# Two squared tiles per chunk in two halves, the low part as the third pass, and T3 ahead of y

## The reference, cut to what matters

```python
# attention: pooled keys/values, softmax, weighted sum -> x (12288 tokens x 128)
# layer 1 (128 -> 2048 -> 128)
h = x @ w_in1; r = np.maximum(h, 0.0); g = r * r
x2 = g @ w_out1
# layer 2 (128 -> 2048 -> 128)
h = x2 @ w_in2
P = a[0] + a[1]*h + a[2]*h**2 + a[3]*h**3
Q = 1.0 + np.abs(b[0])*np.abs(h) + np.abs(b[1])*h**2
out = (P / (Q + 1e-06)) @ w_out2
```

## Time and profile before

| | |
|---|---|
| median of 3 runs | 1517.82 us (1517.7 to 1518.0) |
| profiled execution, its own time | 1517.89 us |
| its span | 1515.9 us |
| granted TensorE clock, mean | 1.0 |
| PE, DVE, ACT, POOL busy | 98%, 95%, 91%, 82% |

### The profile page before, as it was taken

How to read it: one execution, slowest core, us unless ns; L and a number is a source line. 1 busy time by engine, 2 the same in 40 slices (tenths; PEclk the granted TensorE clock), 3 DMA queues, 4 the chain that set the end, 5 groups by cost and what they waited for, 6 DMA issues and landing times.

```text
span 1515.9 us, 20584 instructions
## 1 busy us (share of the span) xinstructions
PE 1483.7 (98%) x5576; PEld 991.1 (65%) x5576; DVE 1445.2 (95%) x2549; ACT 1378.8 (91%) x2672; POOL 1248.3 (82%) x1225
## 2 busy tenths in 40 slices
PE   5999999999999999999999999999999999999988
PEld 4999999765666666666666666666666666666655
DVE  7888888889999999999999999999999999999998
ACT  3777777689999999999999999999999999999997
POOL 4544445359999999999999999999999999999897
PEclk9999999999999999999999999999999999999999
DMA  6200001000000000000000000000000000000000
GB/s 224 84 21 28 21 27 43 1 1 1 8 8 8 1 8 8 8 8 1 7 8 8 0 8 8 8 1 8 7 8 1 8 8 8 8 1 8 8 8 7
DMA packets 11518, 24.21 MB, mean 16 GB/s; under 512 B 1440, under 2 KB 2336, under 8 KB 11168
## 3 DMA queue, kind: packets, MB, share of 16 engines
q1 hardware_dynamic: 11424, 23.14, 4.5%
HBM read 16.85 MB, written 6.29 MB: 15 GB/s over the span
## 4 chain that ended last, share of the span: by engine, by line
PE 88%; DVE 5%; ACT 2%; POOL 2%; issue 1%; DMA 1%; SPq 0%; POOLq 0%; ACTq 0%; DVEq 0%
PE psum L937 19%; PE psum L974 18%; PE psum L801 11%; PE psum L800 11%; PE psum L802 11%; PE psum L889 6%; PE psum L852 6%; PE psum L874 4%; DVE tb L727 1%; DVE tb L736 1%; DVE tb L753 1%; DVE g1h L713 1%; DVE psum L741 1%; POOL tb L410 1%; DMA X<-kvT 1%
## 5 line engine op out<-in xcount | busy, mean ns | idle before, releaser
L412 POOL TENSOR_TENSOR wb<-wb,ub 128x512 f32<-128x512 f32 x384 | 496.4, 1293 | 29.4
L937 PE MATMUL psum<-tb,wout 128*128 128x512 f32 x736 | 375.8, 592 | 2.5 <-DVE tb L785 2.3
L974 PE MATMUL psum<-g,wout 128*128 128x512 f32 x690 | 352.4, 592 | 0.2 <-ACT x2f L528 0.2
L404 POOL TENSOR_SCALAR wb<-ub,babs 128x512 f32<-128x512 f32 x384 | 296.0, 771 | 35.5 <-ACT ub L550 30.3
L800 PE MATMUL psum<-x2h,win2h 128*128 128x512 f32 x384 | 283.3, 738 | 2.6 <-POOL x2l L397 2.5
L727 DVE SCALAR_TENSOR_TENSOR tb<-tb,ca,psum 128x512 f32<-128x512 f32 x364 | 267.8, 736 | 4.6 <-ACT psum L584 4.5
L736 DVE SCALAR_TENSOR_TENSOR tb<-tb,ca,psum 128x512 f32<-128x512 f32 x365 | 269.6, 739 | 0.0
L551 ACT ACTIVATE tb<-psum,ca 128x512 f32<-128x512 f32 x384 | 267.1, 696 | 0.0
L550 ACT ACTIVATE ub<-psum 128x512 f32<-128x512 f32 x384 | 233.0, 607 | 23.5 <-PE psum L802 23.5
L568 ACT ACTIVATE lnb<-wb 128x512 f32<-128x512 f32 x384 | 248.3, 647 | 5.2 <-POOL wb L412 4.8
L753 DVE SCALAR_TENSOR_TENSOR tb<-psum,tb 128x512 f32<-128x512 f32 x364 | 248.1, 682 | 2.6
(11 more groups left out here) (109 smaller groups left out, 2506.6 us busy)
## 6 DMA issues: line engine op xcount, KB each, us to landing
qraw<-qT SPq DMA_DIRECT2D x23, 256.0 KB, 2.6
outT<-osb SPq DMA_DIRECT2D x23, 256.0 KB, 2.0
X<-kvT SPq DMA_DIRECT2D x15, 384.0 KB, 7.7
wraw<-w_in SPq DMA_DIRECT2D x2, 1024.0 KB, 8.3
X<-kvT SPq DMA_DIRECT2D x2, 192.0 KB, 10.5
outT<-osb SPq DMA_DIRECT2D x2, 128.0 KB, 1.8
qraw<-qT SPq DMA_DIRECT2D x1, 192.0 KB, 10.2
wsr<-w_sr SPq DMA_DIRECT2D x1, 64.0 KB, 1.8
```

The source lines that it names most:

```text
L404: nc.gpsimd.tensor_scalar(w, u, babs[:, 1:2], babs[:, 0:1], ALU.mult, ALU.add).then_inc(v_rdy, 1)
L412: nc.gpsimd.tensor_tensor(w, w, u, ALU.mult).then_inc(w_rdy, 1)
L937: mm(ACC2, wout2[:, f, :], tb[:, t % T_RING, :], start=(f == 0), stop=(f == NF - 1))\
L974: mm(ACC1, wout1[:, f, :], g1[:, t % G_RING, :], start=(f == 0), stop=(f == NF - 1))\
```

## The change

Four edits. `SPLIT_COLS` gets column 5, so that two tiles per chunk go through the three-pass form: on each added tile PE does three fp32r passes in place of the f32 matmul, ACT makes one more high half (step 6) and POOL one more low half (end of step 5). POOL's `x1_high` moves from step 5 to step 6 and `x1_low` from step 5 to step 8. In `in2` and in `out1` of halved tiles the pass that reads the low part of the moving operand becomes the third, and the wait for that part stands right before it. On DVE, T3 (tile s-20) is issued ahead of y (tile s-21), except where POOL makes the T2 that T3 reads; both loops share this order.

```diff
-        SPLIT_COLS = (13,)
+        SPLIT_COLS = (5, 13)
...
             for s in range(STEPS):
-                if s % NF == 5 and 1 <= s // NF < NCH - 1:
+                if s % NF == 6 and 1 <= s // NF < NCH - 1:
                     x1_high(s // NF + 1)
+                if s % NF == 8 and 1 <= s // NF < NCH - 1:
                     x1_low(s // NF + 1)
...
-            for s in range(TAIL_S):
-                t = s - LAG - 2
+            def make_y(t):
+
                 if in_b(t):
                     y, r = tb[:, t % T_RING, :], h2(t)
                     dve.wait_ge(r_rdy, t + 1)
                     nc.vector.scalar_tensor_tensor(out=y, in0=y, scalar=ca[:, 0:1], in1=r,
                                                    op0=ALU.add, op1=ALU.mult).then_inc(y_rdy, 1)
-                t = s - LAG - 1
+
+            def make_t3(t):
+
                 if in_b(t):
                     p = tb[:, t % T_RING, :]
                     if by_pool(t):
@@ -735,6 +738,14 @@
                         dve.wait_ge(t2_rdy, t + 1 - pool_t2(t + 1))
                     nc.vector.scalar_tensor_tensor(out=p, in0=p, scalar=ca[:, 1:2], in1=h2(t),
                                                    op0=ALU.add, op1=ALU.mult).then_inc(t3_rdy, 1)
...
+            for s in range(TAIL_S):
+                if by_pool(s - LAG - 1):
+                    make_y(s - LAG - 2)
+                    make_t3(s - LAG - 1)
+                else:
+                    make_t3(s - LAG - 1)
+                    make_y(s - LAG - 2)
...
             for s in range(TAIL_S, STEPS):
-                t = s - LAG - 2
-                if in_b(t):
-                    y, r = tb[:, t % T_RING, :], h2(t)
-                    dve.wait_ge(r_rdy, t + 1)
-                    nc.vector.scalar_tensor_tensor(out=y, in0=y, scalar=ca[:, 0:1], in1=r,
...
+                if by_pool(s - LAG - 1):
+                    make_y(s - LAG - 2)
+                    make_t3(s - LAG - 1)
+                else:
+                    make_t3(s - LAG - 1)
+                    make_y(s - LAG - 2)
...
                     if t % NF == 0:
-                        pe.wait_ge(*((x2l0_rdy, 1) if c == 0 else (x2_rdy, c)))
+                        pe.wait_ge(x2h_rdy, c + 1)
...
-                    three(h2(t), win2h[:, f:f + P], win2l[:, f:f + P],
-                          x2h[:, c % 2, :], x2l[:, c % 2, :]).then_inc(h2_rdy, 1)
+                    mm(h2(t), win2h[:, f:f + P], x2h[:, c % 2, :], start=True, stop=False)
+                    mm(h2(t), win2l[:, f:f + P], x2h[:, c % 2, :], start=False, stop=False)
+                    if t % NF == 0:
+                        pe.wait_ge(*((x2l0_rdy, 1) if c == 0 else (x2_rdy, c)))
+                    mm(h2(t), win2h[:, f:f + P], x2l[:, c % 2, :], start=False, stop=True).then_inc(h2_rdy, 1)
...
                         pe.wait_ge(sqh_rdy, n + 1)
+                        mm(ACC1, wo1h[:, f, :], g1h[:, n % 2, :], start=(f == 0), stop=False)
+                        mm(ACC1, wo1l[:, f, :], g1h[:, n % 2, :], start=False, stop=False)
                         pe.wait_ge(sql_rdy, n + 1)
-                        three(ACC1, wo1h[:, f, :], wo1l[:, f, :], g1h[:, n % 2, :], g1l[:, n % 2, :],
-                              start=(f == 0), stop=(f == NF - 1)).then_inc(g1_used, 1)
+                        mm(ACC1, wo1h[:, f, :], g1l[:, n % 2, :], start=False, stop=(f == NF - 1)).then_inc(g1_used, 1)
```

## The result

The changed kernel takes 1525.55 us (median of 6 runs, 1525.02 to 1525.88), the kernel before 1517.92 us in runs beside it (1517.7 to 1518.12). The ratio is 1.005, 95% interval 1.0037 to 1.0063: slower by 7.6 us. Forecast was slower by 4.2 us, with a range that ended at 1525.2; the time lies 0.35 us above it.

A forecast was written before the change was run, and what follows sets the result against it. PE bounds the kernel before; after the change a loop over ACT and POOL does, at 49.91 us a chunk. 5.1 us for the chunks, less 0.4 and 0.5, give +4.2: 1522.0 us, forecast's own range 1519.5 to 1525.2, overall from 1513.3.

The forecast's parts named there:

- the sum behind the loop: Whole kernel: 21 rounds x 0.25 = 5.3 us, 5.1 with chunk 23, less 0.4 and 0.5 at the ends: +4.2 us.
- the last loop: Where the last loop opens, Exp waits 0.6 us for T3 once; T3 first takes 0.5 us off, between 0 and 0.6.
- the way in: Start of layer 2, before the 21 counted rounds: the prediction's sum has no term for it.
- a loop over ACT and POOL: Steady chunks: POOL's bursts delay ACT and ACT delays POOL, without PE; 49.91 us a chunk against PE's 49.50 and today's 49.66.
- four crossings: Where the round passes between ACT and POOL: into POOL at v(5) and v(13), back to ACT at Ln(11) and Ln(15).
- The stretches of the loop: One chunk's round from Abs(5): 21.00 us to Ln(11), 4.61 to Abs(13), 7.44 to Ln(15), 16.86 to Abs(5); together 49.91.
- The opening: Where layer 2 opens, two passes run before the wait for x2l: 0.4 us off, between 0 and 0.5.
- PE's saving: Each of 23 new halved tiles takes PE 0.15 us less, 3.5 us in all; PE's own work becomes 49.50 us a chunk.
- The first: Rival: PE stays the bound in the steady part, and 4.4 us come off, giving 1513.5 us; chance 0.15.
- Rival 3: More than the loop: PE stalls for x2l or out1 too, some 0.15 us a chunk more, 1525 us; chance 0.05.
- Rival 2: The loop lands near today's pace, 49.6 to 49.75 us a chunk, giving 1516 to 1519 us; chance 0.20.
- Rival 4: The halved tiles save PE nothing; given no chance of its own.

The follow-up runs named there:

- split5_only: The kernel before with column 5 halved as well and nothing else changed; x1_high and x1_low both stay at step 5: 1526.03 us, ratio 1.0053.
- no_split5: The changed kernel with column 13 alone halved; the move of x1_high and x1_low, the pass order and T3 first stay: 1516.82 us, ratio 0.9993.
- x1_at_3_7: The changed kernel with x1_high at step 3 instead of 6 and x1_low at step 7 instead of 8: 1514.46 us, ratio 0.9978.
- x37_y_first: The kernel x1_at_3_7 with the old order on VectorE, y ahead of T3, in both loops: 1515.59 us, ratio 0.9985.
- third_only: The kernel before with the low part as the third pass and its wait behind the first two passes, nothing else: 1517.56 us, ratio 0.9998.

## Why the prediction was right in kind and short in size

**The step that failed is the sum behind the loop: 21 rounds at 0.25 us, nothing for the way into them, and 0.5 us off for the last loop.** The mechanism held. The two profiles in stretches, read from ACT's Abs (L550 and L551; the numbers are tiles of layer 2):

| stretch | before, us | changed, us | difference | forecast |
|---|---|---|---|---|
| start to the first Abs | 320.33 | 319.92 | -0.4 | -0.4 |
| tile 0 to 16, the way in | 48.78 | 50.43 | +1.65 | 0 |
| tile 16 to 352, 21 rounds | 1042.70 | 1049.89 | +7.2 | +5.3 |
| tile 352 to 365 | 39.92 | 39.44 | -0.5 | -0.15 |
| tile 365 to the end | 64.2 | 64.1 | 0 | -0.5 |
| together | 1515.9 | 1523.8 | +7.9 | +4.2 |

A round costs 0.34 us more and not 0.25, which gives 1.9 of the 3.7 us missing between the profiles (3.4 between the medians). With the measured rounds and the rest as forecast the sum would be 1524.0 us, still within the range; the 1.65 us of the way in and the 0.5 us that didn't come off take it past 1525.2. The prediction's text also gives 1525.5 and 1525.2 us for one and the same loop of 50.06 us; its own sum gives 1525.2.

*Who becomes the bound: right.* That a loop over ACT and POOL overtakes PE was the forecast, and the runs show it from both sides: shorten POOL's low half, or take the cast out of its way, and 11 us come back; shorten ACT's high half and little comes back. In the changed kernel its four crossings are where they were put: v(5), Ln(11), v(13), Ln(15). The reason given for them was only half of it: split5_only has the same pace with the split of x ahead of v(5) and the loop over other crossings, of which the runs show Ln(7) and not the rest.

*The stretches of the loop: each right to 0.05 us, the whole to 0.1.* Abs(5) to Ln(11) was forecast as 21.00 us and is 946.98 - 925.97 = 21.01. Ln(11) to Abs(13): 4.61 and 951.60 - 946.98 = 4.62. Abs(13) to Ln(15): 7.44 and 909.08 - 901.59 = 7.49. Ln(15) to Abs(5): 16.86 and 925.97 - 909.08 = 16.89. Together 49.91 and 50.01. One term was off, though its stretch doesn't show it: Abs to v at step 5 is 0.83 us and not 0.73, since Abs lasts 0.73 us there. The durations on ACT grow while it runs without a pause, 0.59 at step 0 to 0.73 at step 5; I had taken 0.63. g1l to x1_high, 1.22 where I had 1.26, and others gave it back; that this stretch came out at 21.01 is luck in part. What the sum lacks is spread over the other stretches, in hundredths.

*The way in: put at nothing.* I counted 21 rounds from the first split to the last and nothing for the way in. From the first Abs of layer 2 to the seventeenth the changed kernel takes 50.43 us, the kernel before 48.78 (both from the starts on ACT's timeline): 1.65 us more. no_split5 has everything but the second halved tile and takes 48.93, so 1.50 us of it come with that tile. From 320 to 370 us PE's weight load waits for DVE's G in both kernels (4.5 us in 11 waits, then 6.8 in 12), so PE isn't the one that sets the pace there. That work added to ACT and POOL therefore counts at once, without slack, is argued and not tried. x1_at_3_7 takes 49.88 in the same place. The 13 tiles ahead of the last loop gave 0.5 us back (39.92 and 39.44 us), where I had allowed 0.15.

*The last loop: the saving is there, the total isn't shorter.* I took off 0.5 us because Exp waited for T3 there. In the chain of waits of the changed kernel, 1455 to 1475 us, T3 (L739), now first, releases what x2h stands behind:

```profile
1463.38 0.67 DVE tb L739
...
1464.60 0.58 ACT x2h L527
```

But from the Abs of tile 365 to that of tile 383 the changed kernel takes 51.99 us and the kernel before 52.05. With y first it would have been longer: split5_only takes 52.71, and x37_y_first, which differs from x1_at_3_7 (51.83) in the order alone, 52.73. So T3 first brings 0.7 to 0.9 us (split5_only differs in the move and the pass order too), and the kernels with the second halved tile lose 0.4 to 0.7 us at the same place against those without it (no_split5: 51.46). The long rounds can't be the whole cause, since x37_y_first and x1_at_3_7 haven't got them. What it is stays open.

*The opening*: 0.4 us earlier, as forecast (first Abs at 319.9 where the kernel before has 320.3), though by one profile each: kernels with the same opening have it from 319.7 to 320.7. *The third pass and T3 first cost nothing*: right, by their own runs. *PE's saving*: right, 0.15 us a halved tile, hidden here and paid out in x1_at_3_7, where 21 rounds take 49.48 us each against 49.65. *No wait for the third pass to remove*: the weight load had one for x2l, 8.7 us in all, but it cost nothing, as third_only shows.

*The rivals.* The first, PE stays the bound at 1513.5 us, was wrong for this change but is what the same edits give with x1_high elsewhere, 1514.5 us. I had said that it decides by 0.4 us in one stretch; it is decided by 0.5 (50.01 against 49.5), and the 0.6 us of the cast cross that line. Rival 3, PE enters the loop again at 1525 us, came nearest by its number and is wrong by its mechanism: PE's weight load does wait for x2f and x2l, but from 480 to 1400 us ACT has no wait for PE, so PE's stalls don't come back into the loop. Rival 2, today's pace, is out with 50.00 us a round. Rival 4 is out with the 0.15 us that PE saves. The page "Perfetto Trace Analysis" of the Trainium skill, section "Identifying the Most-Contended Engine", has the engine with the highest occupancy optimized first. Taken by the busy shares alone that pointed at PE, though the same section says that matmul busy time is not a good measure of how close TensorE is to its roofline: the relief is real there, and worth something only where the engine that pays for it has the time at that place. POOL was the least busy of the four at 82% and became half of the bound.

## What to carry to other kernels

When work is handed to an engine with idle time, don't compare the sum of its waits with the work: find the place where a later engine needs its result, and add up the queue from the last wait in front of it. Where two in-order engines wait for each other, add start-to-start distances round one period through the crossings; if that exceeds the period of today's bound, the time is the loop's. Then look which instruction between two crossings needn't be there: moving a 0.6 us cast out of the longest stretch, to a step ahead of POOL's wait at v(5), turned 7.6 us lost into 3.3 us won (ratio 0.9977), and the instruction next to the longest wait didn't have to move. And count a loop from where it starts: the way into it took 1.65 us of its own.

## What the runs showed of the hardware

In these traces an ACT instruction's recorded duration grows while the engine runs without a pause, and falls back after a wait: Abs of the same tile shape lasts 0.59 us at 910.61, right after a wait, and 0.73 us at 925.97, five steps later, while the distance to the next instruction's start stays the same, 0.48 us. What waits for its result sees the longer one: v starts 0.83 us behind the start of that Abs, and 0.71 behind one of 0.61 us (901.59 to 902.30). POOL's distances between instructions that didn't wait were the same in both kernels to within 0.05 us.
